# A new prologue, an earlier read of the rank bank, and a loop written out, in a fused attention + MLP + mixture-of-experts kernel

## The reference

```python
# attention, per token t
y[:, :, t] = einsum('bhd,bhde->bhe', rt, state + einsum(u * kt, vt))
state = wt[..., None] * state + einsum('bhd,bhe->bhde', kt, vt)
# first MLP: w_in 384 x 2048, w_out 2048 x 384, leaky slope alpha
h = x @ w_in; g = maximum(h, 0) + alpha * minimum(h, 0); x = g @ w_out
# mixture of experts: 8 experts, the best one per token, width 1024
logits = x @ w_gate; e = argmax(logits); p = softmax(logits)[e]
out = p * (maximum(x @ w1[e], 0) @ w2[e])
```

## Time and profile before

| quantity | value |
|---|---|
| median of three runs | 898.5 us |
| profiled execution | 896.84 us |
| its span | 895.0 us |
| TensorE matmul busy | 773.5 us (86%) |
| weight load busy | 474.0 us (53%) |
| VectorE busy | 471.2 us (53%) |
| GpSimd busy | 426.1 us (48%) |
| ScalarE busy | 411.9 us (46%) |
| mean DMA rate | 160 GB/s |
| mean granted TensorE clock | 0.944 |

### The profile page before, as it was taken

How to read it: one execution, slowest core, us unless ns; L and a number is a source line. 1 busy time by engine, 2 the same in 40 slices (tenths; PEclk the granted TensorE clock), 3 DMA queues, 4 the chain that set the end, 5 groups by cost and what they waited for, 6 DMA issues and landing times.

```text
span 895.0 us, 17258 instructions
## 1 busy us (share of the span) xinstructions
PE 773.5 (86%) x5639; PEld 474.0 (53%) x5640; DVE 471.2 (53%) x974; ACT 411.9 (46%) x756; POOL 426.1 (48%) x386
## 2 busy tenths in 40 slices
PE   4744999899899897989989999916999999999992
PEld 2322666566566564656656665503555555555551
DVE  7687667668647664757667534122333333333330
ACT  3745766646547554647647655512232222222220
POOL 5376668758759656659659755720010100101000
PEclk9977999999989998989999999966999999999997
DMA  9465354355355342453462323986353114514110
GB/s 353 189 261 184 137 212 161 126 201 181 119 197 191 134 171 98 169 206 119 170 221 102 133 104 128 332 316 221 144 189 145 61 53 170 192 36 172 50 37 14
DMA packets 42720, 143.15 MB, mean 160 GB/s; under 512 B 4864, under 2 KB 16928, under 8 KB 40864
## 3 DMA queue, kind: packets, MB, share of 16 engines
q1 hardware_dynamic: 30016, 119.19, 37.2%
q10 hardware_dynamic: 9120, 12.93, 5.3%
q0 software_dynamic: 3520, 10.17, 2.9%
HBM read 99.27 MB, written 43.78 MB: 160 GB/s over the span
## 4 chain that ended last, share of the span: by engine, by line
PE 45%; POOL 19%; issue 17%; DMA 8%; DVE 6%; ACT 3%; ACTq 0%; POOLq 0%; SPq 0%; DVEq 0%
POOL arena L548 6%; DMA arena<-expert_split 5%; PE bank L1634 4%; PE bank L1636 4%; PE bank L1635 4%; PE bank L1601 4%; PE bank L1602 3%; PE bank L1603 3%; POOL act_buf L554 3%; PE bank L1488 3%; PE bank L1490 3%; PE bank L1489 3%; PE bank L1476 2%; PE bank L1477 2%; PE bank L1479 2%
## 5 line engine op out<-in xcount | busy, mean ns | idle before, releaser
L554 POOL TENSOR_TENSOR act_buf<-act_buf 128x384 f16<-128x384 f32 x128 | 122.6, 958 | 156.8 <-ACT act_buf L750 155.6
L1117 DVE SCALAR_TENSOR_TENSOR act_buf<-neg,slope,bank 128x384 f32<-128x384 f32 x128 | 78.0, 610 | 158.5 <-ACT neg L743 157.9
L643 POOL DMA_INDIRECT out_dram<-shared,dest x28 | 27.5, 983 | 264.3 <-DVE shared L1337 264.3
L1476 PE MATMUL bank<-xh,arena 128*128 128x384 f16 x384 | 127.8, 334 | 18.4 <-DVE prod L936 12.7
L743 ACT ACTIVATE neg<-bank 128x384 f32<-128x384 f32 x128 | 62.6, 489 | 150.6 <-PE bank L1479 148.7
L1488 PE MATMUL bank<-arena,act_buf 128*128 128x392 f16 x384 | 130.0, 339 | 2.0 <-POOL act_buf L554 1.9
L1490 PE MATMUL bank<-arena,act_buf 128*128 128x392 f16 x384 | 130.1, 339 | 0.0
L1489 PE MATMUL bank<-arena,act_buf 128*128 128x392 f16 x384 | 130.0, 339 | 0.0
L1477 PE MATMUL bank<-xl,arena 128*128 128x384 f16 x384 | 127.1, 332 | 0.0
L548 POOL TENSOR_TENSOR arena<-arena 128x768 f16<-128x768 f32 x64 | 108.9, 1701 | 0.0
L1479 PE MATMUL bank<-xh,arena 128*128 128x384 f16 x384 | 84.4, 329 | 0.0
(11 more groups left out here) (158 smaller groups left out, 1581.1 us busy)
## 6 DMA issues: line engine op xcount, KB each, us to landing
arena<-w_exp_dram SPq DMA_DIRECT2D x32, 768.0 KB, 6.0
expert_split<-arena SPq DMA_DIRECT2D x32, 768.0 KB, 4.1
arena<-expert_split SPq DMA_DIRECT2D x8, 3072.0 KB, 10.6
rk_sb<-rk_in_dram SPq DMA_DIRECT2D x24, 512.0 KB, 5.1
tok<-rk_tok_dram SPq DMA_DIRECT2D x24, 384.0 KB
route_rows<-pad_rows ACTq DMA_DIRECT2D x8, 788.0 KB, 8.1
w_sb<-w_dram SPq DMA_DIRECT2D x24, 256.0 KB, 6.2
shared<-route_rows ACTq DMA_DIRECT2D x31, 197.0 KB, 2.8
```

What stands on the lines that cost most here:

```text
L554: pool.tensor_tensor(gl[:, f % 4, :], gf[:, f % 4, :], gh[:, f % 4, :], ALU.subtract).then_inc(gl_done, 1)
L1476: pe.matmul(at, wih[:, k, fs], xh[:, half, k, :], start=(k == 0), stop=False)
```

## The change

- Prologue. The order of loads and of every engine's steps is new: the attention of the first half comes first. A fourth staging buffer `wide_more` holds a piece of w_out. ScalarE makes one pass per piece (scale and round at once), and all four low parts are made on VectorE by one instruction with the scale in it. The gate columns are computed by `gate_cols`: 128x128 tiles of w_out_t are the weights and the 8 columns of w_gate move (24 matmuls per piece, two pieces); the copies and transposes are gone. The second piece of w_in and of w_out and the decays of the next half's chunks 1 and 2 move into the first half (f = 0 to 6). In the prologue the even inverses are made by GpSimd (`inverses_even`).
- First half. The eight `unit_high` run at f = 8 to 15 instead of from f = 5 on, `unit_low` at 9 to 15 instead of 5 to 10. `hidden` f = 0 no longer waits for decays.
- Rank bank. `place_rows` now also updates `next_row`, counts a new semaphore `rank_evac`, and stands right behind `low_x` at f = 10; `scores` waits for `rank_evac`. `place_chosen` (the multiplication) stays where it was.
- The loop over batches 1 and 2 is written out on all five engines.

```diff
-            load_v(0, 0, 0, True)
             load_tok(0, 0, 0, True)
-            sp.dma_start(wide[2], w_out_t[0]).then_inc(wide_in[2], 16)
+            load_v(0, 0, 0, True)
             load_w(0, 0, 2)
-            load_v(0, 0, 1, True)
             sp.dma_start(wide[0], w_in[0]).then_inc(wide_in[0], 16)
             load_rk(0, 0, 2)
             load_tok(0, 0, 1, True)
-            sp.dma_start(wide[1], w_in[1]).then_inc(wide_in[1], 16)
+            load_v(0, 0, 1, True)
+            sp.dma_start(wide[2], w_out_t[0]).then_inc(wide_in[2], 16)
...
+            sp.wait_ge(wide_free[1], 1)
+            sp.wait_ge(wide_free[0], 2)
             load_hu(0, 0)
             load_hu(0, 1)
...
-            with sp.Fori(1, B - 1) as b:
+            for b in range(1, B - 1):
...
+            def inverses_even(b, half, c):
+                m, at = 6 * b + 3 * half + c, (half + c) % 2
+                pool.wait_ge(odd_done, m + 1)
+                every_second = inv[:, at, :].rearrange("p (j r) -> p j r", r=2)
...
             def w_in_high(i):
-                act.wait_ge(wide_in[i], 16)
-                act.activation(wide[i], wide[i], ACT.Copy, scale=WIS).then_inc(wide_scaled, 1)
-                act.wait_ge(wide_scaled, 1 + i)
-                act.activation(first_w_in(i, wih), wide[i].rearrange("p (k n) -> p k n", k=KD), ACT.Copy
+                act.wait_ge(wide_in[i], 16 * (i + 1))
+                act.activation(first_w_in(i, wih), wide[i].rearrange("p (k n) -> p k n", k=KD), ACT.Copy, scale=WIS
...
             def place_rows(g):
                 dve.wait_ge(rank_ready, g + 1)
+                if g > 0:
+                    dve.wait_ge(rank_evac, g)
                 dve.tensor_tensor(place[:, :, :], b_y[:, RANK:RANK + NC * NE].rearrange("p (j e) -> p j e", j=NC),
...
+                dve.wait_ge(row_full, 3 * g + 1)
+                dve.tensor_tensor(next_row[:, :], b_y[:, RANK + NC * NE:RANK + (NC + 1) * NE], next_row[:, :], ALU.add
+                                  ).then_inc(rank_evac, 1)
...
+                        if start and f == 0:
+                            w_out_low(0)
+                        if start and f == 1:
+                            inverses(nb, nh, 1)
+                            row_sums(nb, nh, 0)
+                        if start and f == 2:
+                            w_in_low(1)
+                        if f == (3 if start else 1):
                             inverses(nb, nh, 2)
...
+                        if not start and f == 10:
+                            place_rows(g - 1)
...
+                    if start and f == 6:
+                        w_out_low(1)
...
-                if f == 0 and not last_half:
+                if f == 0 and not first and not last_half:
                     pe.wait_ge(scan_done, NC * (g + 1) + 2)
...
                                     if c == 2 and not start:
-                                        pe.wait_ge(row_full, 3 * g - 1)
+                                        pe.wait_ge(rank_evac, g)
...
+            def gate_cols(i):
+                pe.wait_ge(wide_in[2 - i], 16)
+                wt = wide[2 - i].rearrange("p (k f) -> p k f", k=KD)
                 for f in range(8):
                     at = NE * (8 * i + f)
+                    for k in range(KD):
+                        last = pe.matmul(b_gt[:, at:at + NE], wt[:, k, f * 128:(f + 1) * 128], wg_sb[:, k, :],
+                                         start=(k == 0), stop=(k == KD - 1))
                 last.then_inc(gc_turned, 1)
```

More of the change, by code:

```diff
@@ L555, in hidden_low @@
                                    ).then_inc(gl_done, 1)
[L557 to L561, removed]
             pool.wait_ge(const_in, 32)
[L564 to L567, removed]
+            for c in range(2):
+                inverses_even(0, 0, c)
+                decayed_k(0, 0, c)
+                decayed_q(0, 0, c)
             row_products(0, 0, 0)
             row_weights(0, 0, 0)
+            inverses_even(0, 0, 2)
             decayed_k(0, 0, 2)
@@ L572, in _ @@
             diagonal(0, 0, 0)
[L573 to L578, removed]
+            for c in range(1, NC):
+                row_products(0, 0, c)
+                row_weights(0, 0, c)
+                diagonal(0, 0, c)
+            inverses_even(0, 1, 0)
             decayed_k(0, 1, 0)
             decayed_q(0, 1, 0)
-            wide_low(1, first_w_in(1, wih), first_w_in(1, wil), hi_done, 2)
-            wide_low(0, woh[:, 0:8, 0:DM], wol[:, 0:8, 0:DM], hi_done, 3)
             row_products(0, 1, 0)
             row_weights(0, 1, 0)
-            decayed_k(0, 1, 1)
-            decayed_q(0, 1, 1)
             def body(b, first, last):
@@ L597, in body @@
                             unit_low(g - 1, 6)
-                        if not end:
+                        if start:
+                            if f == 1:
+                                decayed_k(nb, nh, 1)
+                            if f == 2:
+                                decayed_q(nb, nh, 1)
+                            if f == 3:
+                                decayed_k(nb, nh, 2)
+                            if f == 4:
+                                decayed_q(nb, nh, 2)
+                        elif not end:
                             if f == 1:
@@ L631, in _ @@
             body(0, True, False)
-            with pool.Fori(1, B - 1) as b:
+            for b in range(1, B - 1):
                 body(b, False, False)
@@ L847, in _ @@
             body(0, True, False)
-            with act.Fori(1, B - 1) as b:
+            for b in range(1, B - 1):
                 body(b, False, False)
@@ L938, in decays, with inverses @@
                 last.then_inc(scan_done, 1)
-            def inverses(b, half, c):
+            def inverses(b, half, c, even=True):
                 m, at = 6 * b + 3 * half + c, (half + c) % 2
@@ L949, in inverses @@
                 dve.tensor_scalar(pend[:, c, :], prod[:, c, :, C], 1.0 / G, None, ALU.mult).then_inc(pend_done, 1)
+                if not even:
+                    return
                 dve.wait_ge(odd_done, m + 1)
@@ L1163, in mlp @@
                             row_sums(b + 1, half, 0)
+                    if start and f == 15:
+                        dve.wait_ge(dve_const, 3)
                     if not start and not end:
@@ L1255, in _ @@
             gate_cols_low()
-            decays(0, 1, 1, b_y[:, 0:C])
-            inverses(0, 1, 1)
-            row_sums(0, 1, 0)
-            dve.wait_ge(dve_const, 3)
             dve.wait_ge(slope_done, 1)
             body(0, True, False)
-            with dve.Fori(1, B - 1) as b:
+            for b in range(1, B - 1):
                 body(b, False, False)
@@ L1267, in _ @@
                 step(2 * B - 1)
+            dve.wait_ge(rank_evac, 2 * B)
             chain = [0]
@@ L1560, in _ @@
             body(0, True, False)
-            with pe.Fori(1, B - 1) as b:
+            for b in range(1, B - 1):
                 body(b, False, False)
```

179 lines of the change are left out of this document (78 added, 101 removed).

## The result

The changed kernel takes 893.1 us (median of 7 runs, 890.5 to 897.3) against 899.3 us for the kernel before beside it (7 runs, 896.3 to 901.3): a ratio of 0.9933, 95% interval 0.9906 to 0.996. It is faster by 6 us where 44 were forecast, and outside the range of 842 to 871. The profiled execution has a span of 889.7 us and a mean granted clock of 0.936 (before: 895.0 and 0.944).

A forecast was written before the change was run, and what follows sets the result against it. Phase one was taken as bound by TensorE, the first 85 us by waits. Prologue net 13.6, rank bank 23.2 and loop 7.6 sum to 44.4 us off 896.84: 852.4, or 854.0 on the median's scale; range 842 to 871.

The forecast's parts named there:

- Rank bank: Second to seventh half: scores no longer waits on VectorE's L1097; gain 23.2 us, bounds 10 to 30.
- I take no: At attend in the rank-bank halves: the new 2.1 us wait on att_low was taken not to lower TensorE's clock.
- Rival B: Rank bank: attend waits longer for att_low and the clock falls, 10 of 23.2 us; 867 us; chance 0.13.
- Loop: Jump back of batches 1 and 2: 5.45 us of issue and slow matmuls go; gain 7.6 us, bounds 5 and 8.
- Rival C: Loop: the issue gap is a code fetch that written-out code has too; 861.6 us; chance 0.08.
- Gate columns: Prologue: 2 x 24 f32 matmuls of 8 columns replace 14.1 us of TensorE, taking 4.4 and 3.6 us.
- The walk: Prologue's step-by-step chain: attend 1 from 27.0, gate piece 1 from 32.4 to 36, hidden at 41.5, turn_k at 66.5 us.
- Rival A: Prologue: two or three steps late, or squeezed splits stall TensorE; only 2 of 13.6 us remain; 865.6 us; chance 0.17.
- w behind the expert loads: Second chunk's attend: decays' load queues behind expert loads on SP; attend 25.1 us after turn_k, costing 3.5 us.
- The squeezed splits: First half, f = 8 to 15: eight splits fill GpSimd's last four steps, covered by two steps' lead; 1 us lost.
- Rival D: Written-out code: never-repeated code must be fetched and stops TensorE, 7.6 us each; eight stops give 915 us; chance 0.03.

The follow-up runs named there:

- e1: The kernel before with only the rank-bank part (place_rows moved behind low_x), loops and prologue as before: 878.8 us, ratio 0.9807.
- e4: The kernel before with the rank-bank part and the written-out loop, old prologue kept: 868.2 us, ratio 0.9682.
- e7: The changed kernel with gate columns from one of three k slices, so tokens are routed by other numbers: 877.7 us, ratio 0.9789.
- e9: e8 with two gate tiles moved behind turn_x of the third chunk and the second piece's high and low parts ahead of the masks: 856.9 us, ratio 0.9558.
- e6: The changed kernel with staging buffers of the second w_in and w_out pieces exchanged, expert loads and splits earlier: 869.1 us, ratio 0.9693.
- e5: The changed kernel with GpSimd's low parts of the expert weights in the first half at f = 8 to 13: 872.8 us, ratio 0.9744.
- e2: The kernel before with only the loop over batches 1 and 2 written out: 888.4 us, ratio 0.9909.
- e8: e6 with gate columns cut around attention steps and behind the first hidden tiles, w_in's second low part at f = 4: 863.0 us, ratio 0.9642.

## Why the prediction was wrong

*Rank bank: right in mechanism, somewhat too high.* 17.4 us by the ratio and 18.6 by the marks of e1, forecast 23.2 (bounds 10 to 30). In the halves with a forecast of 3.8, 4.3, 4.3 and 1.4 us the marks give 3.9, 4.1, 3.5 and 1.3; in the two with 4.7, only 3.1 and 2.7. There the answer "I take no", on whether the new wait of 2.1 us lowers the clock, failed. These windows of the third half of the changed kernel stand around its `attend`:

```profile
268.00:270.00 2.00, 0.46 (x9) 0.46 (x9) 1.48 (x4) 0.00 (x0) 2.00 (x3) 1.00 1.02 409
270.00:272.00 2.00, 2.00 (x33) 1.81 (x29) 0.00 (x0) 1.54 (x2) 0.40 (x1) 0.70 1.02 419
272.00:274.00 2.00, 2.00 (x8) 0.95 (x7) 1.08 (x2) 2.00 (x7) 0.98 (x2) 0.50 0.63 245
```

TensorE was busy 0.46 of 2 us, and the clock fell for some 3 us behind it. e1 shows the same at its third half (granted clock 0.71, 0.50 and 0.94 in the windows of 2 us from 250 to 256, behind a wait of 2.22 us); what is missing from full speed in these windows is 1.7 us, an estimate that covers the 1.6 us short (4.7 - 3.1). The same wait of 2.22 us at 128.38 in the changed kernel was followed by a clock of 1.00, so the length of the wait alone doesn't decide. Rival B holds there with 3.6 us in all (4.7 + 4.7 - 3.1 - 2.7), not 13.

*Loop.* 8.2 us alone against 7.6: right for the kernel before, wrong inside the change, where 3.7 were left. Rival C is out: the gap is absent from e4 and from the changed kernel. The Trainium skill (Runtime: NRT & Kernel Launch, Instruction fetch mechanics) says that a taken branch must fetch its target first when that lies outside the fetched window. The traces agree in that the gap and the instruction transfers stand at the jump back and the gap goes with the loop; the rule has no size, so it doesn't tell 5.4 from 2.1 us.

*Gate columns: the first step that failed.* The forecast put 4.4 + 3.6 us, with an upper bound of 6.7 a piece; 7.29 and 10.25 were measured. The bound was taken from a row that the prediction calls four f32 matmuls of 128 columns, 1.12 us at the low clock, 280 ns each. But that row (L1416, `turn_k`) is four transposes, `pe.transpose`, each listed once, where an f32 matmul is listed twice: another operation, and no ceiling for a matmul. The nearest true row was the one in the earlier trace rows of `attend`'s f32 matmul, with weights of 128x128 and 96 columns moving. Its neighbours in the kernel before, at the full clock, and in the changed kernel, at a granted clock of 0.50, show how long TensorE takes to the next matmul:

```profile
257.06 0.44 PE L1450 MATMUL bank<-st,shared 128*128 128x96 f32 x2
257.34 0.19 PE L1454 MATMUL bank<-vh,att_h 128*128 128x48 f16 x1
```
```profile
108.45 0.71 PE L1456 MATMUL bank<-st,shared 128*128 128x96 f32 x2
108.95 0.25 PE L1460 MATMUL bank<-vh,att_h 128*128 128x48 f16 x1
```

That is 0.28 and 0.50 us, so 6.7 us a piece at the full clock and 12.0 at the low one, an estimate of 13.4 to 24 us for both pieces that would have held (17.5): 24 matmuls of 8 columns cost 427 ns each at the low clock (10.25 / 24). And the clock was assumed to be nearly full, for an engine never idle; the rows show it at 0.50.

The Trainium skill (TensorE: Matmul & The Clock Gate, LDWEIGHTS) gave 107 ns per load of 128 columns, from which the prediction estimated 5.1 us for 48. Its page FP8 and Floating Point Precision (TensorE Precision Notes) says that a true f32 matmul makes four passes through the array. Taking one load per pass, an estimate from the two pages is 427 ns per matmul and 20.5 us for 48. The 427 ns are what is measured at the low clock, and the whole took 17.5 us with a part of it at the full one; the trace lists two loads per matmul, so that there are four of them is not shown.

*The order around them.* The walk had each piece end before its `attend` was due. With the true size they did not: `attend` of the second chunk began at 32.3 (walk: 27.0) and of the third at 49.5 (walk: 36). `hidden` was 15.4 us late, 9.5 of them from the size (17.5 - 8.0), `turn_k` 14.9. The other 5.9 us are not divided up by any run; a granted clock of 0.50 from 29 to 57 us, in everything TensorE does there, is the likely cause (its share is argued, not shown). Rival A named this ("two or three steps of a 25 us walk come late") and priced it at 11.6 us for the whole prologue. e7 and e9 show cause and size: with a third of the columns, or the same columns in the gaps, `turn_k` comes at 70.9 and 69.6, near the forecast 66.5. (e9 holds e6 too, but e6 by itself leaves `turn_k` at 81.86.)

*w behind the expert loads.* Right: `attend` of the second chunk 26.1 us after `turn_k` (107.53 - 81.39; forecast 25.1) and 3.55 us of wait (forecast 3.5). Whether such a wait lowers the clock was a guess between the forecast's rows of 2.58 and 3.87 us; it did (granted clock 0.50 from 108 to 112 us). In e6 1.84 us of the wait are left.

*The squeezed splits: the second step that failed.* The forecast set 15.9 us of GpSimd against 11.8 of TensorE, "covered by two steps of lead; 1 us if not quite". Between 107.5 us and the first mark the changed kernel takes 85.8 us, the kernel before 64.7 (from 107.31). I had weighed GpSimd's work against TensorE's, and it fits. What I left out is that each pair of low parts releases a store, a load and a `unit_high`, with 5.7 us from the load's issue to ScalarE's start (123.51 to 129.20). Rival A had "the squeezed splits stall TensorE" and so was right in kind, with 2 of 13.6 us remaining as its price; the ring alone cost more than all of the 13.6 (e5 undoes it and gains 17.0).

The account: first mark 34.9 us later than forecast (14.9 to `turn_k`, 1.0 to `attend`, 19.0 in the ring and behind it), 3.0 less gained from the first mark to the seventh, and 1.8 us lost from the seventh to the eighth (37.8 against 35.9), together 39.7, where the median missed by 39.1. That 1.8 varies from -0.9 to +1.5 us against 35.9 in e1 to e9 and wasn't pursued.

*Rival D* (written-out code stops TensorE) is out: e2 and e4 are faster than the kernels with a loop.

## What to carry to other kernels

When a change packs work into later steps, don't only weigh the work of each engine against the time: list for each moved piece what it releases (here store, load, and a ScalarE step that stands ahead of others in its order) and walk that ring once around with the latency of the transfer in it. An operation form that no row shows needs a bound from the nearest row of the same operation, at the low clock too: see in the kernel's source what the line of the row really is, since a transpose and a matmul look alike in the rows. And cut a long block on an in-order engine to fit into its waits, rather than put it whole ahead of a step whose operands may be there already.

## What the runs showed of the hardware

- TensorE can be issued without a gap and have half its clock: 5.00 of 5.00 us busy at a granted clock of 0.50, in f32 matmuls of 8 moving columns. In the changed kernel the first piece had a clock of 1.00 from 26 to 28 us, 0.72 in the next microsecond and 0.50 from 29 on, with TensorE busy all the time. In e8 the second piece began at 1.00 and the clock fell while it ran (first row 55 to 60, second 60 to 65 us):

```profile
55.00:60.00 5.00, 5.00 (x47) 4.10 (x47) 5.00 (x3) 3.05 (x4) 0.62 (x2) 1.00 0.00 0
60.00:65.00 5.00, 4.61 (x29) 4.51 (x28) 4.98 (x10) 1.69 (x5) 3.77 (x4) 0.64 0.38 124
```

- An f32 matmul with 128x128 weights and 8 moving columns costs 231 ns at the full clock and 427 ns at half of it (e7). With 96 moving columns it is 0.28 and 0.50 us. So twelve times the moving columns add 17 to 21%: most of the price is that of the weights, and it follows the clock.
- The issue gap of the same hardware loop was 5.4 us with one prologue ahead of it and 2.1 to 2.2 us with another, with two and one instruction transfers at it.
- A GpSimd multiplication of 128x384 (L536) took 3.87 us where it fell beside one of VectorE's long low parts (41.78 us, beside a pass of 3.35 us from 41.62), and 0.83 us at 127.19, beside none of them. The Trainium skill (SBUF — State Buffer, SBUF: two separate sides) says that a VectorE instruction with two SBUF inputs and a GpSimd instruction that reads SBUF lock each other out: whichever starts first holds the shared ports for its whole instruction. The rows agree: both have two inputs in SBUF, VectorE starts first, and the GpSimd operation ends 0.68 us after it.
